# Bucketed attention and two expert layers on one core: GpSimd's order around the row statistics, the first head's order, and two row-max chunks per head split into halves

## What is computed

```python
q_bits = (einsum('bhsd,dk->bhsk', q, proj) > 0); k_bits likewise
q_bucket = sum(q_bits * powers); k_bucket = sum(k_bits * powers)
mask = q_bucket[..., :, None] == k_bucket[..., None, :]
scores = scale * matmul(q, k^T);  scores = where(mask, scores, -1e9)
scores = scores - max(scores);    attn = exp(scores)
attn = attn / (sum(attn) + 1e-09);  x = matmul(attn, v)     # then heads side by side: 1536 x 512
h = x @ w_in; g = max(h, 0) + alpha * min(h, 0); x = g @ w_out            # layer 1, d_ff 2048
h = x @ w_in; P = a0 + a1 h + a2 h^2 + a3 h^3
Q = 1 + |b0||h| + |b1| h^2; out = (P / (Q + 1e-6)) @ w_out                # layer 2
```

## Time and profile before

| | |
|---|---|
| median of three runs | 798.24 us (794.5 to 799.77) |
| the profiled execution | 799.15 us, its span 797.3 us, TensorE clock 0.998 of full |
| busy share of the span | PE 97%, PEld 73%, DVE 65%, ACT 45%, POOL 38% |
| busiest groups | acc L1375 and ps_h L1343, the matmuls of the layers: 31% each of the chain that ended last |

### The profile page before, as it was taken

The page is one execution under the profiler, slowest core; times in us unless marked ns, Lnnn a source line. Parts: engine busy times, 40 slices in busy tenths (PEclk is TensorE's granted clock), DMA queues, the critical chain, the costliest instruction groups (busy, mean ns, idle before and its releaser), DMA issues.

```text
span 797.3 us, 11723 instructions
## 1 busy us (share of the span) xinstructions
PE 775.7 (97%) x3820; PEld 583.7 (73%) x3820; DVE 517.8 (65%) x806; ACT 358.3 (45%) x588; POOL 304.9 (38%) x357
## 2 busy tenths in 40 slices
PE   8889999999989999999999999999999999999998
PEld 5456565666656778888888888887888888888886
DVE  6776676776751654435333533379888988888886
ACT  7434554555544311112011210167766767676673
POOL 7566776776856689200000177781000000000000
PEclk9999999999999999999999999999999999999999
DMA  4666675675571243000000033330000100000001
GB/s 127 169 153 161 165 199 151 165 203 150 139 187 48 78 139 122 28 1 1 0 1 14 1 106 93 92 93 1 2 0 1 53 0 1 1 27 27 1 1 53
DMA packets 34207, 58.86 MB, mean 74 GB/s; under 512 B 9900, under 2 KB 13780, under 8 KB 34164
## 3 DMA queue, kind: packets, MB, share of 16 engines
q1 hardware_dynamic: 31796, 53.15, 24.3%
q10 hardware_dynamic: 2368, 5.15, 2.6%
HBM read 29.59 MB, written 3.24 MB: 41 GB/s over the span
## 4 chain that ended last, share of the span: by engine, by line
PE 75%; POOL 8%; issue 4%; DVE 4%; SPq 3%; DMA 3%; ACT 1%; POOLq 0%; DVEq 0%; ACTq 0%
PE acc L1375 31%; PE ps_h L1343 31%; PE ps_o L590 3%; PE ps_a L505 2%; PE ps_s L560 2%; PE ps_s L565 2%; POOL lo L866 1%; PE ps_o L612 1%; POOL p_sum L873 1%; DMA work<-rden_scratch 1%; POOL pen L882 1%; DMA q<-stats 1%; PE ps_a L501 1%; POOL x_lo L964 1%; DMA raw<-in_qk 1%
## 5 line engine op out<-in xcount | busy, mean ns | idle before, releaser
L1408 ACT ACTIVATE g_hi<-num 128x512 fp32r<-128x512 f32 x96 | 59.9, 624 | 207.2 <-PE acc L1375 203.1
L1478 DVE TENSOR_TENSOR g_lo<-num,g_hi 128x512 fp32r<-128x512 f32 x96 | 71.7, 747 | 78.2 <-ACT g_hi L1408 77.7
L1040 DVE TENSOR_REDUCE row_max<-ps_a 128x1 f32<-128x384 f32 x180 | 92.1, 553 | 40.0 <-PE ps_a L505 37.6
L736 ACT ACTIVATE p<-ps_s 128x768 f32<-128x768 f32 x96 | 77.5, 810 | 67.7 <-PE ps_s L565 64.2
L1343 PE MATMUL ps_h<-x_hi,w_late_in_hi 128*128 128x512 f32 x288 | 78.9, 395 | 1.2 <-POOL w_late_in_lo L1307 1.2
L1343 PE MATMUL ps_h<-x_hi,w_late_in_lo 128*128 128x512 f32 x288 | 78.8, 394 | 0.0
L1343 PE MATMUL ps_h<-x_lo,w_late_in_hi 128*128 128x512 f32 x288 | 78.8, 394 | 0.0
L590 PE MATMUL ps_o<-p,v_use 128*64 128x384 f32 x384 | 74.4, 507 | 0.0
L1486 DVE TENSOR_SCALAR num<-ps_h,alpha_sb 128x512 f32<-128x512 f32 x48 | 36.0, 750 | 54.4 <-PE ps_h L1343 53.7
L1416 ACT ACTIVATE den_q<-ps_h,abs_b 128x512 f32<-128x512 f32 x48 | 33.0, 688 | 83.8 <-PE ps_h L1343 77.6
L1343 PEld LDWEIGHTS ps_h<-x_hi,w_late_in_hi 128*128 128x128 f32 x288 | 53.9, 187 | 14.0 <-POOL w_late_in_lo L1307 1.7
(11 more groups left out here) (167 smaller groups left out, 1569.9 us busy)
## 6 DMA issues: line engine op xcount, KB each, us to landing
stage<-in_w_in SPq DMA_DIRECT2D x26, 256.0 KB, 2.7
stage<-in_w_out SPq DMA_DIRECT2D x26, 256.0 KB, 2.7
raw<-in_qk SPq DMA_DIRECT2D x15, 384.0 KB, 3.0
q<-hi SPq DMA_DIRECT2D x30, 192.0 KB
k<-hi SPq DMA_DIRECT2D x30, 192.0 KB
v_raw<-in_v SPq DMA_DIRECT2D x16, 192.0 KB, 3.0
work<-rden_scratch SPq DMA_DIRECT2D x16, 192.0 KB, 3.3
out<-y SPq DMA_DIRECT2D x12, 256.0 KB, 2.5
```

Source lines behind the costliest of these rows:

```text
L736: nc.scalar.activation(halves(p[c][:]), ps_s[c % 2][:, :, 0:HALF], ACT.Exp, scale=float(D) ** -0.5).then_inc(s_exp, 1)
L1040: dve.tensor_reduce(row_max[slot][:, i, c:c + 1], ps_a[:, i, 0:HALF], AX.X, ALU.max).then_inc(s_a_free, 1)
L1408: nc.scalar.activation(g_hi[f % 2][:], num[f % 4][:], ACT.Copy).then_inc(s_ghi, 1)
L1478: dve.tensor_tensor(g_lo[f % 2][:], num[f % 4][:], g_hi[f % 2][:], ALU.subtract).then_inc(s_glo, 1)
```

## The change

1. **Halves.** `scores` takes a list of halves and makes them between `scores_one` and `scores_two`. In heads 1 to 13 the second half of step 2's chunk is made inside the scores of step 3, and the first half of step 4's chunk inside the scores of step 4. The order in which DVE sees the halves stays.
2. **GpSimd.** `x_low` moves from the end of the odd head to the next even head, behind `row_stats`. `split_weights(0)` and `(1)` move behind `bit_rows` and `split_qk`. The loop starts at pair 2.
3. **SP.** `stage_early(2)` moves from head 12 to the end of head 13.
4. **Head 0.** The bits of head 3 are made behind `turn` instead of ahead of it; head 1's first scores come behind `values` of step 4; ACT's `split_qk` comes one step earlier.

```diff
@@ uses_of, first head
-                            ([("a", 1, 5)], [("bits", 3, 0)]),
-                            ([("m", 1, 0)], [("a", 2, 0)]),
+                            ([("a", 1, 5)], []),
+                            ([("m", 1, 0)], [("bits", 3, 0), ("a", 2, 0)]),
@@ SP's pair
-                        if left == 1 and u == 0:
-                            stage_early(2)
                         if u == 0 and not first:
                             spread(sp, j - 1)
+                        if left == 1 and u == 1:
+                            stage_early(2)
@@ TensorE's scores
+                def scores(slot, jj, c, t, halves=()):
...
                     scores_one(slot, c)
+                    for half in halves:
+                        use(*half)
                     if c == 0:
                         pe.wait_ge(s_stat, 16 * (g + 1))
                     scores_two(slot, c)
@@ TensorE's pair
+                                places = 0, 1
+                                if not first and c == 4:
+                                    places = 1,
+                                    for kind, g, cc in steps[c][0]:
+                                        halves.append((kind, (u + g) % 2, j + (u + g) // 2, cc, n, b, (0,)))
+                                if not first and c == 2:
+                                    places = 0,
                                 if c + 2 < KC:
-                                    scores(u, j, c + 2, t + 2)
-                                elif not (final and u == 1):
-                                    scores(1 - u, j + u, c + 2 - KC, t + 2)
+                                    scores(u, j, c + 2, t + 2, halves)
+                                elif not (final and u == 1 or first and c == 4):
+                                    scores(1 - u, j + u, c + 2 - KC, t + 2, halves)
+                                halves = []
+                                if not first and c == 2:
+                                    for kind, g, cc in steps[c][0]:
+                                        halves.append((kind, (u + g) % 2, j + (u + g) // 2, cc, n, b, (1,)))
...
                                 values(u, h, c, KC * h + c)
+                                if first and c == 4:
+
+                                    scores(1, 0, 0, c + 2)
@@ ScalarE's pair
-                            if c == (4 if first and u == 0 else 2) and (left > 1 or (left == 1 and u == 0)):
+                            if c == (3 if first and u == 0 else 2) and (left > 1 or (left == 1 and u == 0)):
                                 split_qk(1 - u, j + 1 + u)
@@ GpSimd's pair
-                        if final and u == 0:
+                        if u == 0 and not (isinstance(j, int) and j < 2):
                             x_low(j - 2)
                         if not (first and u == 0):
                             add(1, h)
-                        if first and u == 1:
-                            split_weights(0)
-                        if left == 1 and u == 0:
-                            split_weights(1)
...
                             split_qk(1 - u, j + 1 + u)
                         if first and u == 0:
                             add(1, h)
-                        if u == 1 and left > 1 and not first:
-                            x_low(j - 1)
+                        if first and u == 1:
+                            split_weights(0)
+                        if left == 1 and u == 0:
+                            split_weights(1)
```

18 lines of the change are left out of this document (10 added, 8 removed).

## The result

The changed kernel takes 791.0 us (median of 20 runs, 786.81 to 795.97), the kernel before took 798.08 us beside it (20 runs, 793.94 to 801.26): a ratio of 0.9917 with a 95% interval of 0.9898 to 0.9936. That is 0.8% less: 6.6 us by the ratio, 7.1 us between the two medians. I had forecast 786.7 us, 11.5 us less; the measured time lies in the range of 781.5 to 794, but its gain is a little more than half of mine, and by the bound of 1% that I had set it counts as "within 1%", to which I gave 0.23. The profiled execution spans 791.9 us where that of before spanned 797.3, 5.4 us less, at a TensorE clock of 0.994 (before: 0.998). One of all executions in this document, one of e1 (844.12 us at a mean clock of 0.851), is left out of the ratios as a run in a slower state.

A forecast was written before the change was run, and what follows sets the result against it. PE's pace plus its stalls was taken as the bound ahead of the layers. Pieces 59.1 + 139.7 + 16.2 + 13.1 + 43.2 + 514.4 made 785.7 us, 11.6 less than before; forecast 786.7 us, range 781.5 to 794.

The forecast's parts named there:

- A: Whole kernel: the forecast itself, with an error of some us in either direction, 783 to 790 us; chance 0.57.
- C: Loop heads: the halves only move the wait, statistics slip 0.3 us a head in 11 heads, 790 to 793 us; chance 0.19.
- The head at PE's pace: Loop, turn 2 to 12: without row-max stalls and with `x_low` moved, a head takes 13.9 us, two heads 27.8.
- elsewhere: DVE's `p_sum`: 2.47 and 3.50 us in heads 0 and 1, but 0.96 us in all other heads.
- DVE later by one reduction: Row-max halves, step 2: the case giving the lower bound, no gain; the upper bound was 0.32 us a stall.
- The first pair: Turn 2 to 4: only `x_lo` taken off the earlier 30.30 us, giving 28.5 us.
- Heads 0 and 1: Start to turn 2: 1.0 us gained by turn 1, `v_raw` landing earlier, turn 2 at 59.1 us instead of 60.66.
- The collision of `v_three`: Ahead of turn 2: about 0.7 us of collision with `p_sum` that may go.
- The weights in head 1: Moved weight instructions end at 54.5 to 55, ahead of the `v_raw` landing, and cost nothing while that DMA is later.
- Head 12: Turn 12 to 13: `lo` waits for `hi`, 16.2 us, 1.4 worse than before, with a 2.3 us stall.
- the variant of A: Ahead of turn 13: the clock may fall behind the new 2.3 us stall, costing 1.7 us, 788.4 us; no separate chance.
- Behind turn 14: Turn 14 to the end: nothing moves relative to that turn, 43.24 and then 514.44 us.

The follow-up runs named there:

- e1: The kernel before with only the halves moved inside the scores, all other orders as before: 796.55 us, ratio 0.9977.
- e9: The changed kernel with GpSimd's `normalise` computing only 128 of its 768 columns: 787.7 us, ratio 0.9884 to the kernel before.
- e3: The changed kernel with `split_weights(1)` moved from the end of head 12 to head 13, ahead of `normalise`: 786.01 us, ratio 0.9856 to the kernel before.
- e5: The changed kernel with the edits of e3 and e4 together: 785.24 us, ratio 0.9847 to the kernel before.
- e12: e5 with `load_raw` in head 1 issued behind `fill_a_pen` instead of ahead of `load_v`: 785.26 us, ratio 0.9848 to the kernel before.
- e11: The changed kernel with `split_weights(0)`, `split_weights(1)` and `stage_early(2)` back where they stood before: 798.08 us, ratio 0.9994 to the kernel before.
- e10: The changed kernel with 11 added matmuls on zeros in TensorE's wait ahead of turn 13: 788.7 us, ratio 0.9894 to the kernel before.
- e4: The changed kernel with one pair of first-layer weight loads issued ahead of the last `store_rows` and `spread`: 788.49 us, ratio 0.9877 to the kernel before.

## Why the prediction was right, and where it was not

**The range held, the forecast of A did not.** 791.0 us lies outside A's 783 to 790 and inside C's 790 to 793, to which I had given 0.19, and C's cause (statistics 0.3 us late in 11 heads) is not what came: five odd heads are 0.44 us longer, and the even ones stay at 13.9. That the result lies between 781.5 and 794 is owed to the width of that range more than to the sum. The sum took 11.6 us off, 1.7 of them for a lowered clock that would not come again, so 9.9 at equal clock. The executions with a mean clock of 0.999 or 1.000, so without a fall, took 787.75 us on average with the change (5 of 20) and 795.39 before (8 of 46): 7.6 us less. Of the 2.3 us between, the collision of `normalise` and `p_sum` explains most (below). The 1.7 us for the clock did not come either: over all executions the change saved 0.4 us of lowered clock.

**The head at PE's pace: right.** Step 2 and 4 without stalls, 13.9 us from even to odd turns: 13.93 in every pair at full clock. The idle time of PE before `turn` in even heads, forecast at no more than 0.2 us, is gone (the window of turn 8 to 10 counts 27.95 us busy of 27.95).

**The odd heads: a term was missing.** The step that failed is the sentence that DVE's `p_sum` takes 0.96 us "elsewhere". I had read it in an even head (161.85). The odd heads of the kernel before, which I had not looked up, say otherwise in four of five (1.56 to 2.40 us, three of them here; head 3 had 0.96):

```profile
111.44 2.40 DVE L1073 TENSOR_TENSOR p_sum<-p 128x768 f32<-128x768 f32 x1
...
141.23 1.82 DVE L1073 TENSOR_TENSOR p_sum<-p 128x768 f32<-128x768 f32 x1
...
170.44 1.76 DVE L1073 TENSOR_TENSOR p_sum<-p 128x768 f32<-128x768 f32 x1
```

There it was hidden behind POOL's late `mcols`; with a head of 13.9 us it is not. It costs 0.44 us a pair, 2.2 us in all, and e9 gives it back; of that, 1.75 us show against my sum, because my 28.5 us for the first pair were 0.6 too many (27.9 in e9). My bound "DVE later by one reduction", which set the lower end of the halves' gain, was of the right size for it, but I took the other end for all 24. So a piece of what C described was in the kernel all along, in the odd heads only.

**The first pair: right but for the clock.** I had 28.5 us from turn 2 to 4; without the lowered clock it takes 28.2 to 28.7 (e3, e5, e12), with it 30.06.

**Heads 0 and 1.** Turn 2 came at 58.46 instead of 59.1. DVE's `p_sum` in head 0 fell from 2.47 to 0.96 us as computed, in head 1 from 3.50 to 1.87. I had turn 2 set by `v_raw`; the row-max chunk ahead of it waited for `ka<-pen` instead, 1.53 us (57.14), and e12 shows that the statistics were hardly earlier. The collision of `v_three` that I said may go did go (55.51, 0.59 us instead of 1.34).

How the port pair was shared in head 1 I had left open. DVE's `p_sum`, ready at 48.81, ended at 50.68, 0.8 us behind the end of POOL's `lo` (48.04 and 1.82), and the weight instruction that POOL issued at 49.82 took 1.33 us instead of 0.62 (210.02). So DVE got the pair first here. That is what the Trainium skill (SBUF — State Buffer, Who interferes with whom) says, that the engine that issues first holds the pair for its instruction and the other blocks; the 79.94 and 79.89 rows above agree with it as well. Two places don't: 50.85, and head 3 of e11, where DVE's `p_sum` had stood since 84.51 and GpSimd's `lo`, started at 85.15 right behind `normalise`, still took its plain 1.83 us; `p_sum` took 3.85. Which engine gets the pair when both stand is not settled here.

**The weights in head 1: mis-sized beside the other parts.** "They cost nothing" held, but with the other parts in place putting them behind `pen` was worth 6 us (e11), by way of SP's list and of a DMA that landed 2.3 us later. I had followed `v_raw` in that list, not `turn_sums` and the stage loads.

**Head 12: right.** 16.09 us against 16.2, and a stall of 2.24 us against 2.3, by the very steps named: `pen` first, `lo` waiting for `hi`, then the weights ahead of the statistics. It was worth avoiding, as e3 shows.

**Head 13: the variant of A came.** The wait for `q<-stats` is gone and the statistics go out at once, but the clock fell behind the new stall instead. I gave that variant 788.4 us inside A without a chance of its own; e3 and e10 speak for the stall as its cause, and without the fall the piece takes 13.06 us (e10), the 13.1 of the sum.

**Behind turn 14: mis-sized at nothing.** "Nothing moves relative to it" overlooked that a wait stood there, at the cut at 282.86 of the earlier trace rows, which the change could lengthen:

```profile
282.86 1.20 PE L1343 MATMUL ps_h<-x_hi,w_late_in_hi 128*128 128x512 f32 x4 [1.22 <-POOL w_late_in_lo L1307]
```

It became 1.76 us and the clock fell: 2.3 us, which e4 gives back.

In one line, for the profiled execution, which had three falls where the median one had about one: of the 6.2 us that it lacks, 1.25 + 1.55 + 1.7 are lowered clocks behind waits, 1.75 the collision of `normalise` and `p_sum`, and the rest small terms of both signs. The chance I gave to "faster by over 1%", 0.72, was too high because I counted one lowered clock as gone and treated a new one as an accident that might follow one stall, while over all traces 16 of 26 places with PE standing 1.8 us or more between starts had one.
